# Pooled attention and two MLPs on one core: attention laid into the loop of the MLPs, turned by Vector

## The reference

```
kv_flat = mean over 4x4 of kv [384, 32, 128]  @ w_sr      -> [768, 128], k = v
s = (q @ k.T) / sqrt(128);  a = exp(s - max);  a /= a.sum() + 1e-9
x = a @ v
h = x @ moe_w_in  [128, 2048];   g = h * clip(h + 3, 0, 6) / 6;   y = g @ moe_w_out
h = y @ moe2_w_in [128, 2048];   g = h if h >= 1, 0 if h <= -1, else (h + 1)^2 / 4
out = g @ moe2_w_out
```

## Time and profile before

| what | value |
|---|---|
| median of 3 runs | 1386.65 us (1385.42 to 1388.87) |
| span of the profiled execution | 1385.0 us |
| instructions | 19432 |
| data moved | 23.48 MB, mean 17 GB/s |
| first scores start | 33.62 us |
| first stage ends, first MLP matmuls alone | about 325 us |

### The profile page before, as it was taken

How to read it: one execution, slowest core, us unless ns; L and a number is a source line. 1 busy time by engine, 2 the same in 40 slices (tenths; PEclk the granted TensorE clock), 3 DMA queues, 4 the chain that set the end, 5 groups by cost and what they waited for, 6 DMA issues and landing times.

```text
span 1385.0 us, 19432 instructions
## 1 busy us (share of the span) xinstructions
PE 1366.2 (99%) x6517; PEld 1144.3 (83%) x6517; DVE 1166.3 (84%) x1286; ACT 1153.9 (83%) x1429; POOL 205.6 (15%) x152
## 2 busy tenths in 40 slices
PE   7999999999999999999999999999999999999998
PEld 6888888887888888888888888888888888888886
DVE  6777777777988888888888888888888888888888
ACT  1677777667889899899989989898998999899896
POOL 0566655451000000000000000000000000000012
PEclk9999999999999999999999999999999999999999
DMA  9000000000000000000000000000000000000000
GB/s 328 24 23 23 23 23 23 23 1 1 0 1 8 8 8 1 8 8 8 0 8 8 8 8 0 8 8 8 8 0 8 8 8 1 7 8 8 9 0 23
DMA packets 10154, 23.48 MB, mean 17 GB/s; under 512 B 1040, under 2 KB 1168, under 8 KB 9872
## 3 DMA queue, kind: packets, MB, share of 16 engines
q1 hardware_dynamic: 10128, 23.14, 4.8%
HBM read 16.84 MB, written 6.29 MB: 17 GB/s over the span
## 4 chain that ended last, share of the span: by engine, by line
PE 94%; DVE 4%; ACT 1%; issue 0%; DMA 0%; ACTq 0%; DVEq 0%
PE ps L704 37%; PE ps L770 36%; PE ps L640 8%; PE ps L616 7%; PE ps L627 4%; DVE probs L492 1%; DVE g_lo L552 1%; PE ps L602 1%; PE ps L791 1%; DVE gate L546 1%; ACT g_hi L424 0%; DMA x_all<-in_kv 0%; ACT pt_hi L336 0%; DVE pt_lo L484 0%; DVE negmax L470 0%
## 5 line engine op out<-in xcount | busy, mean ns | idle before, releaser
L552 DVE TENSOR_TENSOR g_lo<-gate,g_hi 128x1024 fp32r<-128x1024 f32 x384 | 479.5, 1249 | 108.6 <-ACT g_hi L424 108.5
L546 DVE SCALAR_TENSOR_TENSOR gate<-gate,ps 128x1024 f32<-128x1024 f32 x384 | 451.6, 1214 | 2.9 <-ACT gate L407 2.7
L424 ACT ACTIVATE g_hi<-gate 128x1024 fp32r<-128x1024 f32 x384 | 405.9, 1057 | 1.2 <-DVE gate L546 1.2
L770 PE MATMUL ps<-g_hi,w_hi 128*128 128x512 f32 x768 | 299.2, 390 | 0.6 <-DVE g_lo L552 0.6
L770 PE MATMUL ps<-g_lo,w_hi 128*128 128x512 f32 x768 | 299.0, 389 | 0.0
L770 PE MATMUL ps<-g_hi,w_lo 128*128 128x512 f32 x768 | 298.8, 389 | 0.0
L409 ACT ACTIVATE gate<-ps 128x1024 f32<-128x1024 f32 x192 | 197.7, 1030 | 83.0 <-PE ps L704 79.0
L407 ACT ACTIVATE gate<-ps 128x1024 f32<-128x1024 f32 x192 | 195.9, 1020 | 11.5 <-PE ps L704 10.9
L418 ACT ACTIVATE gate<-gate 128x1024 f32<-128x1024 f32 x185 | 195.2, 1055 | 0.0
L283 POOL TENSOR_TENSOR x_lo<-x_all,x_hi 128x512 fp32r<-128x512 f32 x24 | 31.2, 1300 | 936.3 <-ACT x_hi L388 936.3
L770 PEld LDWEIGHTS ps<-g_hi,w_hi 128*128 128x128 f32 x768 | 144.2, 188 | 31.2 <-DVE g_lo L552 1.0
(11 more groups left out here) (64 smaller groups left out, 1620.7 us busy)
## 6 DMA issues: line engine op xcount, KB each, us to landing
x_all<-in_kv SPq DMA_DIRECT2D x12, 512.0 KB, 8.9
q_in<-in_q SPq DMA_DIRECT2D x24, 256.0 KB, 2.6
out<-out_sb SPq DMA_DIRECT2D x24, 256.0 KB, 2.0
w_raw<-in_moe_w_in SPq DMA_DIRECT2D x2, 1024.0 KB, 17.3
probs<-in_w_sr SPq DMA_DIRECT2D x1, 64.0 KB, 12.8
w_raw<-in_moe_w_out SPq DMA_DIRECT2D x2, 0.5 KB, 13.5
```

The costliest lines, as they stand in the source:

```text
L424: nc.scalar.activation(g_hi[:, n % RING, :], gate[:, n % RING, :], ACT.Copy).then_inc(g_hi_done, 1)
L546: nc.vector.scalar_tensor_tensor(out=gate[:, n % RING, :], in0=gate[:, n % RING, :], scalar=6.0 if mlp == 1 else 1.0, in1=hidden, op0=ALU. ...
L552: nc.vector.tensor_tensor(g_lo[:, n % RING, :], gate[:, n % RING, :], g_hi[:, n % RING, :].bitcast(F32), ALU.subtract).then_inc(g_lo_done, 1)
L770: last = nc.tensor.matmul(ps[:, y_bank(mlp, t), :], left[:, cols], right[:, n % RING, toks], start=(p == 0 and e == 0 and a == 0), stop=(p ...
```

## The change

**The attention of tiles 2 to 23 moves into the loop of the MLPs.** Tables give the step of each of its parts: with a period of 16 steps (one tile pair), scores of tile t + 2 stand in steps 0, 2, 4, 6, the turns of its probabilities in steps 8, 10, 12, 14; pieces of tile t + 1's turned probabilities are split in steps 4, 6, 8 and multiplied by the values in steps 8, 10, 12; x is split in step 14; queries of tile t + 3 are turned in step 4. Tile 0 runs ahead of the loop, tile 1 partly, tiles 2 and 3 in the first 16 steps, with tables of their own.

**All turns but those of tiles 0 and 1's probabilities are made by DVE**, which transposes blocks of 32 x 32 in place; the blocks are brought to their places by DMAs: queries are loaded and results stored in runs of 32 elements (4 transfers a tile each), and a tile's probabilities go from `turned_p` to `pt` by 16 transfers of 32 partitions. Keys are stored in an order that fits this.

**Who does what**: results are turned straight from PSUM (`take_results`); the low parts of probabilities and queries move to POOL; x's low part moves to DVE; the low parts are formed in SBUF for whole pieces of 1024 elements. Hidden blocks have two pairs of banks instead of three in the loop, scores and x share the third. The lag of `add_to_y` is 4 instead of 5, that of the split 1 instead of 2.

**Pooling**: two additions on DVE replace each reduction, and keys and values are made in three parts while the rest loads. Queries and weights are loaded in a new order.

```diff
     def group(n):
-        return 0 if slots[n][0] == 1 else 1 + slots[n][2] % 2
+        return 0 if slots[n][0] == 1 else 1
+    BANK_X = 4
-    LAG = 5
-    SPLIT_LAG = 2
+    LAG = 4
+    SPLIT_LAG = 1
+    scored = [(a, r) for a in range(LEAD, TILES) for r in range(SUB)]
+    pieces = [(a, g) for a in range(LEAD, TILES) for g in range(PIECES)]
+    scores_at = {slot(a - LEAD, r): (a, r) for a, r in scored if a > 3}
+    turn_at = {slot(a - LEAD, 4 + r): (a, r) for a, r in scored if a > 3}
+    piece_at = {slot(a - 1, 2 + g): (a, g) for a, g in pieces if a > 2}
+    values_at = {slot(a - 1, 4 + g): (a, g) for a, g in pieces if a > 2}
+    x_at = {slot(a - 1, 7): a for a in range(3, TILES)}
+    turn_q_at = {slot(a - LEAD - 1, 2): a for a in range(5, TILES)}
+    high_q_at = {slot(a - LEAD - 1, 6): a for a in range(5, TILES)}
+    scores_at |= {n: (2, r) for r, n in enumerate((4, 5, 6, 7))}
+    scores_at |= {n: (3, r) for r, n in enumerate((8, 9, 10, 11))}
+    exp_at = {n + 1: ar for n, ar in scores_at.items()}
+    turn_at |= {n: (2, r) for r, n in enumerate((6, 7, 8, 9))}
+    piece_at |= {n: (2, g) for g, n in enumerate((12, 13, 14))}
+            def load_q(a, k=None):
+                if a:
+                    sp.wait_ge(qt_done, a if k is None else a + 2 * k)
+                for b in range(QUADS):
+                    source = q_blocks[a, b] if k is None else q_blocks[bass.ds(2 * k + a, 1), b].rearrange(
+                        "o i g j -> (o i) g j")
+                    sp.dma_start(block_rows(q_in, b), source).then_inc(q_loaded, 16)
+            def move_probs(a, k=0):
+                sp.wait_ge(p_turned, SUB * (a - 1) + 2 * SUB * k)
+                for b in range(QUADS):
+                    for d in range(QUADS):
+                        sp.dma_start(
+                            pt[d * BLK:(d + 1) * BLK, :].rearrange("p (r t f) -> p r t f", r=SUB, t=QUADS)[:, :, b],
+                            turned_p[b * BLK:(b + 1) * BLK, :, d * QK:(d + 1) * QK]).then_inc(p_moved, 16)
+            with sp.Fori(0, (TILES - 8) // 2) as k:
+                for t in (0, 1):
+                    store(t, k)
+                    load_q(t + 7, k)
+                    move_probs(t + 5, k)
+            def period(t, k):
+                for r in range(SUB):
+                    if t + 1 < TILES and r < PIECES:
+                        probs_low(t + 1, r, k)
+                    if t + LEAD < TILES:
+                        normalise(t + LEAD, r, k)
+                if t + LEAD + 1 < TILES:
+                    q_low(t + LEAD + 1, k)
             def step(n, k):
+                if n in x_at:
+                    x_high(x_at[n], k)
+                if n in y_at and y_at[n][0] == 1:
+                    y_high(y_at[n][1], k)
+                if n < SLOTS:
                     gate_input(n, k)
+                if n < SLOTS and slots[n][0] == 2:
+                    gate_square(n, k)
+                if n in piece_at:
+                    probs_high(*piece_at[n], k)
+                if n in high_q_at:
+                    q_high(high_q_at[n], k)
+                if n in exp_at:
+                    softmax_exp(*exp_at[n], k)
                 if SPLIT_LAG <= n < SLOTS + SPLIT_LAG:
                     gate_high(n - SPLIT_LAG, k)
+            def turn_probs(a, r, k):
+                dve.wait_ge(norm_done, SUB * a + r + 1 + 2 * SUB * k)
+                if a > LEAD and r == 0:
+                    dve.wait_ge(p_moved, 16 * QUADS * QUADS * (a - LEAD) + 32 * QUADS * QUADS * k)
+                nc.vector.transpose(turned_p[:, r, :], probs[:, r, :]).then_inc(p_turned, 1)
+            def sum_halves(m):
+                part = kv_sb[:, m * PART:(m + 1) * PART].rearrange("p (g b c) -> p g b c", b=2, c=2 * C)
+                nc.vector.tensor_tensor(part[:, :, 0], part[:, :, 0], part[:, :, 1], ALU.add).then_inc(halves_summed, 1)
+            def take_results(t, k):
+                dve.wait_ge(y_added, slot_of[(2, t, PAIRS - 1)] + 1 + BODY * k)
+                if t:
+                    dve.wait_ge(stored, 16 * QUADS * t + 32 * QUADS * k)
+                nc.vector.transpose(out_sb[:], ps[:, y_bank(2, t), :]).then_inc(out_ready, 1)
             def step(n, k):
+                if n in x_at:
+                    x_low(x_at[n], k)
+                if n in y_at and y_at[n][0] == 1:
+                    y_low(y_at[n][1], k)
+                if n in y_at and y_at[n][0] == 2:
+                    take_results(y_at[n][1], k)
+                if n in scores_at:
+                    row_max(*scores_at[n], k)
+                if n < SLOTS:
                     gate_value(n, k)
+                if n in turn_at:
+                    turn_probs(*turn_at[n], k)
+                if n in exp_at:
+                    invert(*exp_at[n], k)
+                if n in turn_q_at:
+                    turn_q(turn_q_at[n], k)
                 if SPLIT_LAG <= n < SLOTS + SPLIT_LAG:
                     gate_low(n - SPLIT_LAG, k)
             def step(n, k):
+                if n < SLOTS:
                     hidden_block(n, 0, k)
                     hidden_block(n, 1, k)
                 if LAG <= n < SLOTS + LAG:
                     add_to_y(n - LAG, k)
+                if n in values_at:
+                    values(*values_at[n], k)
+                if n in scores_at:
+                    scores(*scores_at[n], k)
```

899 lines of the change are left out of this document (475 added, 424 removed).

## The result

The changed kernel takes 1361.88 us (median, 1360.85 to 1364.19); the kernel before, on the same chip, 1386.79. The ratio is 0.9823, 95% interval 0.9808 to 0.9838: 25 us less, where the forecast said 67. The profiled execution has a span of 1359.4 us.

What follows compares the result with a forecast made beforehand. TensorE's instructions were taken to bound the kernel. Opening 44.5 + kept TensorE work 1232.8 + first-step stall 10 + loop loss 20 x 1.16 + squares 1 + end 6 = 1317.5 us, 1319 as median; range 1298 to 1390.

Steps and rivals of the forecast that it cites:

- 44.5 us for the opening: Opening: first scores at 25, then tile 0's attention alone; first MLP matmul at 44.5 us (41 to 49).
- the 10 of stall in the first steps: First 16 steps: 10 us of stall added (4 to 20), with Vector at some 60 us and TensorE at 58.
- the 51.8 of matmuls in a period: One period of the merged loop: TensorE's work, 192 x 0.227 + 4 x 1.05 + 3 x 1.36 = 51.8 us.
- rival (a): Merged loop: Vector becomes the bound if a turn costs 1.5 us; period 54 to 56, time 1361; chance 0.24.
- gates 4 and 6: Period of the loop: gate 4 ready at 19.9 for 19.7 (0.2 lost), gate 6 at 27.1 for 26.4 (0.7 lost).
- The lock inside it: Loop: Vector's two-SBUF-operand operations wait GpSimd's out; g_lo of steps 3, 5, 7, 8 lose about 0.7, 0.9, 1.0, 0.3 us.
- the walk: Layout of one 16-step loop period, engine by engine: loss of 1.16 us, period 52.9 us.
- 1.05 us for two additions: Opening, pooling of keys: two additions replace each reduction, 12 x 1.05 = 12.6 us, then wait for the loads.
- third by third, so about 5 us of chain follow: Opening: copy, key and split work done by thirds, leaving about 5 us after the loads; first scores at 25.
- 1 for squares: End of the kernel: 1 us added for GpSimd's squares, beside 6 for the finish after the last matmul.
- no wait for a DMA: Sign of a right forecast in the merged loop: placing takes 11 us against 15.3 available, so it stays hidden.
- rival (b): Loop: probabilities arrive late at Scalar's first piece, step 4; slower from 18.5 us of placing, 1418 at 20; chance 0.15.

Runs made afterwards that it cites:

- e3: Changed kernel with the PSUM pairs of the last 16 slots in order 2, 0, 1 instead of 1, 0, 2: 1362.15 us.
- The two experiments, 14 and 16 us: Single edits of the changed kernel: gate before row maximum on Vector, 1347.67 us; GpSimd's products of tiles 2 to 23 cut to 32 columns, 1345.97 us.
- e9: Changed kernel with tile 2's probabilities copied row for row by 4 DMAs instead of placed by 16 (result not the attention's): 1358.4 us.
- e7: Kernel before, with two additions instead of each reduction of the keys and nothing else: 1381.72 us.
- e4: Changed kernel with 2 idle transposes instead of 6 between the pooling's small matmuls for the first two thirds: 1362.13 us.
- e8: Changed kernel, opening only: first q tile's DMAs after all keys, first two key splits on Vector behind later additions: 1362.52 us.
- e11: Changed kernel, opening only: Scalar's rounding of the first piece of weights put after the fourth exponential of tile 0: 1360.93 us.
- e14: Changed kernel with bank pairs 2, 0, 1 in the last 16 steps and GpSimd's seven squares cut to 32 columns: 1354.17 us.
- e17: Changed kernel with gate first, reordered first steps and opening, plus bank pairs 2, 0, 1 at the end, GpSimd squaring every second step: 1343.45 us.
- e6: Changed kernel with each of the 16 DMAs that place a tile's turned probabilities cut in two: 1513.06 us.

## Why the prediction was right and wrong, point by point

It said faster, by 67 us; it is 25. The direction and the removed work were right, nearly every stall outside the loop was sized too small, and in the loop TensorE's own work was. The steps that failed are terms of the sum: 44.5 us for the opening measured 52.46, the 10 of stall in the first steps 21.6, the entry to the loop had no term and cost 3, the end was 8 longer than carried over, and the 51.8 of matmuls in a period are 52.2. Against the sum of 1317.5 us the span is 41.9 longer:

| term of the sum | forecast | measured | difference |
|---|---|---|---|
| first MLP matmul | 44.5 | 52.46 | +8.0 |
| first 16 steps | 67.5 | 79.1 | +11.6 |
| from there into the loop | | | about +3 |
| 18 periods of the loop | 52.9 | 53.54 | +11.5 |
| last interval before the end | 43.6 (192 x 0.227) | 48.5; without the stop, in e3, 44.8 | +4.9 |
| last copy of y to the end | as before, 46.0 | 49.3 | +3.3 |

(The differences are read from single rows and sum to 42.3.)

- **TensorE's work: right in number, a little too cheap.** From the first MLP matmul on, the matmuls of the trace come to 1233.6 us at the prediction's prices; it had 1232.8. But a period without a gap takes 52.34 us (the row above), of which 0.1 is wait, where the sum had 51.8: values, scores and the blocks behind them cost more than the prices taken from the earlier trace rows.
- **Turns: right**, 0.97 for 0.95. So rival (a), whose time the result has, is wrong in its mechanism: it wanted turns of 1.5 and had periods of 54 to 56. That the number fits is chance.
- **The period: right mechanism, right size of the waits, the price of the work too low.** TensorE waits for y's low half and for gates 4 and 6, as laid out: about 0.1, 0.3 and 0.65 us by its starts, for 0.25, 0.2 and 0.7 in the forecast, with one more of 0.1 ahead of gate 4. Against a period free of them (52.34 less 0.1) the measured 53.54 has 1.3 of waits; the forecast was 1.16. So of the 0.6 us a period that the forecast is short, and of its 11.5 over the loop, about three quarters is the term 51.8 for TensorE's matmuls, and the rest is waits.
- **The lock inside it: mis-sized on both sides, with little effect on the sum.** I added GpSimd's delay to Vector, but took GpSimd's own durations as undisturbed. The product is not: 2.46 us for 1.47, so a burst lasts longer and meets another g_lo. And the piece was priced by the wrong row: 1.9 is the square of the earlier trace rows, while a piece takes 2.41 with nothing beside it, up to 3.06 with. The two experiments, 14 and 16 us, show both halves of the walk (row maximum ahead of the gate; exclusion).
- **First 16 steps: outside the stated bounds.** Of the 4 to 20 us of stall I took 10, and 21.6 came. The prediction named that tile 2's rows are wanted three steps after they are turned, but had no term for placing them: 16 DMAs in 11.25 us and 2 to land, 5.1 us too late for Scalar and 5.6 for TensorE, of which e9 took back 3.5. Nor did I see that scores in consecutive steps share one pair of banks with their exponentials (five times 0.62), nor GpSimd's queue ahead of qt_lo (1.6).
- **Entry to the loop: not in the sum.** The same placing, of tile 3, is 3.3 us late for Scalar, and TensorE waits 2.7 us at 157.18. That is nearly all of the 3 us there. No experiment took this wait away.
- **Opening: outside the stated bounds** (41 to 49). 1.05 us for two additions was right (0.69 + 0.42, the second overlapped), and they alone gave 4.7 us (e7). Of the 8.0 us, 6.3 stand ahead of the first scores. The failed step is "third by third, so about 5 us of chain follow": splits placed among the additions held Vector up 4.23 us, first scores came at 31.28 for 25, and behind them a scaling met w_lo (2.23 for 0.5). How much each of these cost in time stays open, since e4, e8 and e11 lie inside the scatter of the opening.
- **The end: one term missing.** I carried the 1.9 us squares and the old 46.0 over as "1 for squares", though the lag of the split had gone from 2 to 1 and that of `add_to_y` from 5 to 4, and the bank of the step ahead of the first of these steps was now the same as its own. The traces of e14 and e17 show some 5.2 us for the squares and 2.2 for the banks.
- **Placing: right in the loop, wrong ahead of it.** It takes 0.64 us for a DMA instead of 0.54, about 12.5 us instead of 11, and is hidden in every period; e6 shows the cliff. But the sign "no wait for a DMA" failed for tiles 2 and 3, as said above: there rival (b)'s mechanism cost some 8 us. The 128-byte runs of queries and results land in 2.2 and 1.8 us for 64 KB, the median of 96 each, and nothing in the loop waits for them. The Trainium skill (DMA: Bandwidth & Descriptors, "Specifications") asks for 512 B at least; no run here shows a cost of breaking that.

## What to carry to other kernels

When a change fills an engine to nine tenths and takes away slack (banks, lags), walk one period for every *kind* of step, the start, the entry to the loop and the end included: here these cost 31 of the 42 us that the forecast was short, and the 18 periods 11.5. Put the instruction that frees the bottleneck's buffer (the gate) ahead of what waits on the bottleneck's last work (the row maximum). And price two engines that exclude each other in both directions: the burst that delays you also gets longer by you. Take a duration from a row of the same operation and not only of the same size: the square's 1.9 us stood for a subtraction of 2.41.
